# Laying the weights of a fused attention and two-MLP kernel out differently, matrix by matrix

## The reference

```python
# q, k, v: (1, 6016, 256); tau = 1
qn = q / (norm(q, axis=1) + 1e-06);  kn = k / (norm(k, axis=1) + 1e-06)
s = kn.transpose(0, 2, 1) @ qn / tau           # (1, 256, 256)
a = softmax(s, axis=-1)
x = (v @ a).reshape(6016, 256)
# first MLP, 1536 hidden units
g = x @ w_gate;  val = x @ w_val               # (256, 1536) each
x = (g * sigmoid(g) * val) @ w_out             # (1536, 256)
# second MLP, 2048 hidden units
h = x @ w_in2                                  # (256, 2048)
out = (h * clip(h + 3, 0, 6) / 6) @ w_out2     # (2048, 256)
```

## Time and profile before

| what | value |
|---|---|
| median of 2 runs | 1173.93 us (1173.82 to 1174.04) |
| the profiled execution's own time | 1172.61 us |
| its span in the profile | 1170.8 us |
| granted TensorE clock, mean | 0.996 of full speed |
| PE busy / PEld busy | 1156.0 / 972.5 us |
| VectorE / ScalarE / GpSimd busy | 718.0 / 286.7 / 80.6 us |

### The profile page before, as it was taken

How to read it: one execution, slowest core, us unless ns; L and a number is a source line. 1 busy time by engine, 2 the same in 40 slices (tenths; PEclk the granted TensorE clock), 3 DMA queues, 4 the chain that set the end, 5 groups by cost and what they waited for, 6 DMA issues and landing times.

```text
span 1170.8 us, 14739 instructions
## 1 busy us (share of the span) xinstructions
PE 1156.0 (99%) x5274; PEld 972.5 (83%) x5274; DVE 718.0 (61%) x1162; ACT 286.7 (24%) x456; POOL 80.6 (7%) x47
## 2 busy tenths in 40 slices
PE   8899999999999999999999999999999999999998
PEld 7788888888888888888888888888888888888998
DVE  5788664574575485475476466466557447548555
ACT  7551221212221222122122122122122222212121
POOL 5766000000000000000000000000000000000000
PEclk9899999999999999999999999999999999999999
DMA  9723011002002002002002001000200200100100
GB/s 342 241 91 90 1 18 18 0 0 36 0 0 36 0 0 36 0 0 36 0 0 36 0 0 23 13 0 1 35 0 0 36 0 0 32 0 0 18 2 14
DMA packets 108111, 33.76 MB, mean 29 GB/s; under 512 B 98624, under 2 KB 102464, under 8 KB 108096
## 3 DMA queue, kind: packets, MB, share of 16 engines
q1 hardware_dynamic: 107952, 33.56, 11.6%
q10 hardware_dynamic: 144, 0.00, 0.0%
HBM read 27.39 MB, written 6.16 MB: 29 GB/s over the span
## 4 chain that ended last, share of the span: by engine, by line
PE 97%; issue 1%; DVE 1%; POOL 0%; ACT 0%; POOLq 0%; DVEq 0%; ACTq 0%
PE psum L690 33%; PE psum L667 32%; PE psum L678 22%; PE psum L702 5%; PE psum L567 3%; PE psum L652 1%; PE psum L562 0%; DVE diag_q L455 0%; POOL qk_parts L298 0%; DVE norms L449 0%; PE psum L611 0%; DVE act_out L522 0%; PE psum L621 0%; DVE prod L509 0%; PE psum L615 0%
## 5 line engine op out<-in xcount | busy, mean ns | idle before, releaser
L690 PE MATMUL psum<-prod,down_w 128*128 128x512 f32 (+1 forms) x1728 | 426.8, 384 | 0.0
L690 PEld LDWEIGHTS psum<-prod,down_w 128*128 128x128 f32 x1728 | 322.5, 188 | 61.8
L678 PE MATMUL psum<-yT,up_w 128*128 128x512 f32 (+1 forms) x1152 | 281.4, 385 | 0.0
L678 PEld LDWEIGHTS psum<-yT,up_w 128*128 128x128 f32 x1152 | 215.0, 188 | 41.3
L522 DVE TENSOR_TENSOR act_out<-psum,act_out 128x512 f32<-128x512 f32 (+1 forms) x144 | 97.9, 680 | 237.4 <-PE psum L667 207.0
L667 PE MATMUL psum<-vT,gate_w 128*128 128x512 f32 (+1 forms) x864 | 215.6, 385 | 0.1
L667 PE MATMUL psum<-vT,val_w 128*128 128x512 f32 (+1 forms) x864 | 215.3, 384 | 0.0
L667 PEld LDWEIGHTS psum<-vT,gate_w 128*128 128x128 f32 x864 | 161.2, 188 | 31.7 <-DVE act_out L522 0.8
L667 PEld LDWEIGHTS psum<-vT,val_w 128*128 128x128 f32 x864 | 161.3, 188 | 30.9
L386 ACT ACTIVATE act_out<-psum 128x512 f32<-128x512 f32 (+1 forms) x144 | 85.2, 591 | 394.4 <-PE psum L667 370.8
L535 DVE SCALAR_TENSOR_TENSOR act_out<-act_out,psum 128x512 f32<-128x512 f32 (+1 forms) x192 | 129.0, 672 | 76.8 <-ACT act_out L394 76.7
(11 more groups left out here) (68 smaller groups left out, 355.0 us busy)
## 6 DMA issues: line engine op xcount, KB each, us to landing
qk<-in_q SPq DMA_DIRECT2D x11, 512.0 KB, 4.6
qk<-in_k SPq DMA_DIRECT2D x11, 512.0 KB, 5.9
v_in<-in_v SPq DMA_DIRECT2D x44, 128.0 KB, 3.4
out<-out_sb SPq DMA_DIRECT2D x44, 128.0 KB, 2.5
w_stage<-in_moe_w_out SPq DMA_DIRECT2D x7, 512.0 KB, 3.8
w_stage<-in_moe_w_in SPq DMA_DIRECT2D x4, 512.0 KB, 3.7
raw_up<-in_moe_w_gate SPq DMA_DIRECT2D x3, 512.0 KB, 6.8
raw_up<-in_moe_w_val SPq DMA_DIRECT2D x3, 512.0 KB, 7.6
```

What stands on the lines that cost most here:

```text
L678: end = mm(HID[j % 4][:, 0:n], up2_w[:, part, b, j * P:(j + 1) * P], yT[:, m, b, 0:n], start=(part, m, b) == (0, 0, 0), stop=(part, m, b) ...
L690: end = mm(banks[h][:, 0:n], w[:, part, j, h * P:(h + 1) * P], prod[:, c % 4, m, 0:n], start=j == 0 and (part, m) == PASSES[0], stop=False)
```

## The change

Where the operands of TensorE lie in memory changes, and nothing of what is computed. Tensors keep their sizes in whole multiples of 512 words, apart from the room that the offsets take.

- **Backward tokens in the first MLP.** `up` streams `vT` from the last token to the first, so the hidden units come out in reverse token order; `down` and `finish` of the first MLP stream `prod` backwards too, which puts the tokens in order again.
- **Unit blocks with a stride of 16 in `up2`.** Block j no longer is columns 128j to 128j + 127 of `up2_w` but every 16th column from j on, so each weight load reads 128 words that lie 64 bytes apart. `w_out2` is read as "(p j) c" to match. Since a block now needs columns of all four pieces, TensorE waits once for the last piece of `up2_w` before the first block, in place of a wait at every fourth block.
- **Offsets.** `val_w` begins 16 bytes later, `down_w` 64 bytes later. `down2_w` begins 16 bytes later, is laid out with one half of the channels behind the other, and the second half stands 30 words further, so it is 8 bytes off a multiple of 16.

```diff
+        def moved(name, words, by):
+            return sb(name, [P, -(-(words + by) // BANK) * BANK], fp32r)[:, by:by + words]
...
-        val_w = sb("val_w", [P, 2, KC, F1], fp32r)
+        val_w = moved("val_w", 2 * KC * F1, 4).rearrange("p (m k f) -> p m k f", m=2, k=KC)
...
-        down_w = sb("down_w", [P, 2, J1, C], fp32r)
+        down_w = moved("down_w", 2 * J1 * C, 16).rearrange("p (m j c) -> p m j c", m=2, j=J1)
         up2_w = sb("up2_w", [P, 2, KC, F2], fp32r)
-        down2_w = sb("down2_w", [P, 2, J2, C], fp32r)
+        down2_w = moved("down2_w", KC * (2 * J2 * P + 30), 4).rearrange("p (h x) -> p h x", h=KC)
...
+        def down2(part, blocks, h):
+            return down2_w[:, h, 0:2 * J2 * P].rearrange("p h (m j c) -> p h m j c", m=2, c=P)[:, :, part, blocks, :]
...
+        def down2_pieces(w):
+            view = w.rearrange("(p j) c -> p j c", j=J2)
+            return [(view[:, j:j + 4, :], [down2(part, slice(j, j + 4), slice(0, KC)) for part in range(2)], 4,
+                     lambda ap: ap.rearrange("p j (h c) -> p h j c", c=P)) for j in range(0, J2, 4)]
...
-                            end = mm(HID[(2 * j + g) % 4][:, 0:n], w[:, part, b, j * P:(j + 1) * P], vT[:, m, b, 0:n],
+                            end = mm(HID[(2 * j + g) % 4][:, 0:n], w[:, part, b, j * P:(j + 1) * P],
+                                     vT[:, m, b, 0:n][:, ::-1],
...
-                    end = mm(HID[j % 4][:, 0:n], up2_w[:, part, b, j * P:(j + 1) * P], yT[:, m, b, 0:n],
+                    end = mm(HID[j % 4][:, 0:n], up2_w[:, part, b, j::J2], yT[:, m, b, 0:n],
...
+            def down_block(w, part, j, h):
+                return w[:, part, j, h * P:(h + 1) * P] if w is down_w else down2(part, j, slice(h, h + 1))[:, 0]
+
+            def tokens(w, c, m, n):
+                return prod[:, c % 4, m, 0:n][:, ::-1] if w is down_w else prod[:, c % 4, m, 0:n]
...
-                        end = mm(banks[h][:, 0:n], w[:, part, j, h * P:(h + 1) * P], prod[:, c % 4, m, 0:n],
+                        end = mm(banks[h][:, 0:n], down_block(w, part, j, h), tokens(w, c, m, n),
...
-                pe.wait_ge(w_split, MLP2_AT + 1)
+                pe.wait_ge(w_split, MLP2_AT + 2 * (J2 // 4) - 1)
...
-                        if j % 4 == 0:
-                            pe.wait_ge(w_split, MLP2_AT + 2 * (j // 4) + 1)
```

More of the change, by code:

```diff
@@ L88, in attention_mlp_mlp_kernel @@
         gate_w = sb("gate_w", [P, 2, KC, F1], fp32r)
-        val_w = sb("val_w", [P, 2, KC, F1], fp32r)
+        val_w = moved("val_w", 2 * KC * F1, 4).rearrange("p (m k f) -> p m k f", m=2, k=KC)
         with ExitStack() as early:
             raw_up = sb("raw_up", [P, 2, KC, F1], fp32, early)
+            first_pad = sb("first_pad", [P, BANK], fp32, early)
             first_up = sb("first_up", [P, 2, 2, KC, F1], fp32r, early)
-        down_w = sb("down_w", [P, 2, J1, C], fp32r)
+        down_w = moved("down_w", 2 * J1 * C, 16).rearrange("p (m j c) -> p m j c", m=2, j=J1)
         up2_w = sb("up2_w", [P, 2, KC, F2], fp32r)
-        down2_w = sb("down2_w", [P, 2, J2, C], fp32r)
+        down2_w = moved("down2_w", KC * (2 * J2 * P + 30), 4).rearrange("p (h x) -> p h x", h=KC)
         w_stage = sb("w_stage", [P, 2, 4 * C])
@@ L194, in up_pieces @@
             step = 4 * C // KC
-            return [(view[:, :, n:n + step], dst[:, :, :, n:n + step], KC) for n in range(0, width, step)]
+            return [(view[:, :, n:n + step], [dst[:, part, :, n:n + step] for part in range(2)], KC, lambda ap: ap)
+                    for n in range(0, width, step)]
         def down_pieces(w, dst, blocks):
             view = w.rearrange("(j p) c -> p j c", p=P)
-            return [(view[:, j:j + 4, :], dst[:, :, j:j + 4, :], 4) for j in range(0, blocks, 4)]
+            return [(view[:, j:j + 4, :], [dst[:, part, j:j + 4, :] for part in range(2)], 4, lambda ap: ap)
+                    for j in range(0, blocks, 4)]
+        def down2_pieces(w):
+            view = w.rearrange("(p j) c -> p j c", j=J2)
+            return [(view[:, j:j + 4, :], [down2(part, slice(j, j + 4), slice(0, KC)) for part in range(2)], 4,
+                     lambda ap: ap.rearrange("p j (h c) -> p h j c", c=P)) for j in range(0, J2, 4)]
         PIECES = down_pieces(w_out, down_w, J1)
         MLP2_AT = len(PIECES)
-        second = zip(up_pieces(w_in2, up2_w, F2), down_pieces(w_out2, down2_w, J2))
+        second = zip(up_pieces(w_in2, up2_w, F2), down2_pieces(w_out2))
         PIECES += [piece for pair in second for piece in pair]
@@ L262, in _ @@
             load_v(v_full[0], BANK)
-            for n, (src, _, _) in enumerate(PIECES):
+            for n, (src, _, _, _) in enumerate(PIECES):
                 if n >= 2:
@@ L313, in _ @@
             pool.wait_ge(up_split, 2)
-            for n, (_, dst, _) in enumerate(PIECES):
+            for n, (_, (high, lo), _, read) in enumerate(PIECES):
                 if n == MLP2_AT:
@@ L317, in _ @@
                 pool.wait_ge(w_loaded[n % 2], 16 * (n // 2 + 1))
-                nc.gpsimd.tensor_copy(dst[:, 0], staged(n)).then_inc(w_high, 1)
+                nc.gpsimd.tensor_copy(high, read(staged(n))).then_inc(w_high, 1)
                 pool.wait_ge(w_high, n + 1)
-                nc.gpsimd.tensor_tensor(dst[:, 1], staged(n), dst[:, 0].bitcast(fp32),
-                                        ALU.subtract).then_inc(w_split, 1)
+                nc.gpsimd.tensor_tensor(lo, read(staged(n)), high.bitcast(fp32), ALU.subtract).then_inc(w_split, 1)
         @block.scalar
@@ L701, in finish @@
                         pe.wait_ge(prod_ready, t * JJ + (c + k + 3))
-                    end = mm(banks[h][:, 0:n], w[:, part, j + k, h * P:(h + 1) * P], prod[:, (c + k) % 4, m, 0:n],
+                    end = mm(banks[h][:, 0:n], down_block(w, part, j + k, h), tokens(w, c + k, m, n),
                              start=False, stop=k == 1 and (part, m) == PASSES[-1])
```

## The result

The changed kernel takes 1211.3 us (2 runs, 1211.29 to 1211.32) against 1173.93 us: 1.0318 times as long, 95% interval 1.0274 to 1.0363. That is slower by more than 2%, where a change too small to tell from none was forecast. The time lies in the stated range of 1168 to 1304 us, but by luck: that range reached so far up only to hold loads of three times the length, which did not come, and the forecast's own range ended at 1186 us.

A forecast was written before the change was run, and what follows sets the result against it. TensorE, going gaplessly from matmul to matmul at 226.7 ns, was taken as the bound; 1172.6 + 0 + 1 + 0 + 0 = 1173.6 us profiled, 1174.9 against the median, so 1175 us predicted, range 1168 to 1304 us (the forecast's own 1168 to 1186).

The forecast's parts named there:

- loads of three times the length: In `up2`, strided weight loads at 321 ns would outlast the stream: 129 us more, 1304 us in all.
- The cost of the moved wait: TensorE's wait before `up2` for the last `up2_w` piece: expected 0, the piece being ready 22.1 us ahead.
- I take zero: First MLP's 2592 backward matmuls: no cost, as 16 bytes serve four columns in either direction.
- first rival: Backward streams of the first MLP run at half pace: 542 us more, 1717 us in all; chance 0.13.
- third rival: Many small costs: 5 to 10 ns at each backward stream's start, 13 to 26 us, about 1200 us; chance 0.03.
- The strided load takes 1.69 times as long: `up2` weight loads: VectorE's measured strided-read ratio put on the contiguous 107 ns gives 181 ns; 2 us at most, 1 taken.
- the fixed 13.3 ns: Part of each 226.7 ns matmul step that does not grow with columns; 512 columns take the other 213.5 ns.
- The price given for twice: Strided loads of double length: covered by 512 columns, 96 x 53 ns = 5.1 us in the last tile.
- second rival: Strided `up2` loads outlast their cover, above twice the contiguous length: 1304 to 1426 us; a collision about 105 us; chance 0.17.
- Covered, so no cost in 11 tiles: Strided `up2` loads of 181 ns stay below the 213.5 ns stream of 512 columns: 0 in 11 tiles.
- I take 0: Shifted `val_w`, `down_w`, `down2_w`: same 16-byte groups, 33 for 32 in one half, covered; 1.7 us if uncovered.
- The mark that was set for backward streams: Sign of a wrong forecast: 12 matmuls of a first MLP taking over 2.8 us.

## Where the prediction held and where it failed, step by step

**The frame held.** TensorE bounded the kernel before and after, no engine came into its way, and the growth came from longer steps between matmuls, all but some 0.6 us of the lead-in. The cost of the moved wait stayed at nothing: GpSimd ended the last piece of `up2_w` at 103.8 us, and TensorE came to `up2` at 127.5. The timeline of GpSimd in the changed kernel:

```profile
101.34 2.43 POOL L336 TENSOR_TENSOR up_w<-w_stage,up_w 128x1024 fp32r<-128x1024 f32 x1
```

**"I take zero" for the backward tokens** is the first step that failed. The reason, four words to each 16 bytes in either direction, speaks against the half pace of the first rival, and nothing like it came. It does not exclude a small cost, and there is one: 6.7 ns (1.44 us in 216) on each of 2376 matmuls and 0.7 to 0.9 us in the last tile, 16.6 us measured alone. It is an even one: the mean over an MLP was the same in every full tile but the first of all five kernels with backward tokens, 50.39 to 50.41 us, and 6.7 ns is what 16 columns take at 0.417 ns. The third rival priced 5 to 10 ns a matmul and had 3 of 100. It was nearest in kind and size, and its 13 to 26 us hold the 16.6. Its place, the start of each stream, is not shown: with 384 columns, where as many streams start, the cost was 0.5 to 0.9 us in 216 matmuls, 2 to 4 ns each. The estimate should have asked what a stream without cover pays for any small thing, times 2592.

**"The strided load takes 1.69 times as long"** was mis-sized. The recorded load grew by 114 ns, and in the last tile, where it is bare, the step of 225 ns leaves 212 ns for it, twice the contiguous 107 (an estimate: 225 less the fixed 13.3 ns). The price given for twice, 96 x 53 = 5.1 us, is what the last tile paid (5.1 us). As to the size, VectorE's ratio was no guide to TensorE's, and with a stride of 4 the same estimate gives 220 ns, more than the 213.5 of the cover: there the second rival's condition was met, by a little.

What the Trainium skill says of 16-byte lines (Advanced Engine Details and Errata, section SBUF Cachelines) agrees with the recorded loads of this case: one hit per line made them 302 ns (stride of 16) and 311 ns (4) long, two hits with a stride of 2 kept them at 193 against 188 ns.

**"Covered, so no cost in 11 tiles"** is the step that failed most. It took the load for something that runs beside the stream and matters only once it is longer. The stride of 2 refutes that: a load recorded with 193 ns, covered with 384 columns at next to no cost, and 233 ns a step of `up2` with 512. The full tiles paid 13.9 us for the stride alone. The second rival named a collision of load and stream and was nearer in kind, but priced it at 105 us.

**"I take 0" for the offsets** counted how many 16-byte groups a block touches. By that count 16, 64 and 128 bytes are free and 8 bytes cost a little. Measured: 8 bytes, 256 bytes and, as far as it shows, 16 bytes are free, 128 bytes dear, and 64 bytes too in the one run that has them (there beside 16 on `val_w`). What counts is the place of a block of weights, by itself or against the tokens streamed beside it, and a shift by 256 bytes changed nothing. In the kernel before, all blocks of weights began at multiples of 512 bytes from where the streams begin, so no row of it could show this.

The two independent read ports that the Trainium skill gives TensorE (SBUF — State Buffer, the table under "The single rule") were used against a collision. The measurement decides otherwise as to the time: here the place and the pattern of loads that end well within the stream changed the step by 4 to 7 ns, so that stream and load are not independent in time, whatever couples them.

**The sum.** 233.3 ns in the first MLP and 234.6 in the second, against 226.7 forecast, 32.6 us in 11 tiles, and 5.8 us in the last against 1 forecast. The mark that was set for backward streams, 12 matmuls in over 2.8 us, stood where a cost of this size just reaches it: they took 2 x 1.40 = 2.80 us in the timeline above. And of the third rival's 1188 to 1201 us about seven tenths, not a third, lie within 2% of the kernel before.

**What stays open.** That load and stream meet in the memory is one explanation of the cost of place and of the stride of 2, but no run shows the meeting itself, and short loads, which should meet less, disturbed forward streams in place by 4 and 5 ns. What adds to the stride of 16 in full tiles beyond the length of its load is not known. Whether the place of the weights counts by itself or against the tokens was not told apart. The 233.3 ns of the backward stream hung neither on the place of the weights (0, 16, 64, 128 bytes) nor on the load's length, in five kernels; that it is a cost of the stream itself is the simplest reading, and why it then absorbs the cost of the offsets was not settled. That the half at 136 bytes is what makes the layout of `down2_w` dear is argued from the run with 128 bytes and was not tried by itself.

No version tried beats the kernel before, and no MLP of a full tile got under 226.7 ns a step as a mean.

## What to carry to other kernels

Where TensorE goes from matmul to matmul without a gap, a layout of its operands is a change of every step: ask for the price in nanoseconds per matmul, not whether a load is covered. Begin the blocks of weights and the tokens beside them at the same place within 256 bytes, which was free where all of them stood so (the kernel before, and all tensors 16 bytes later); weights 256 bytes later were free too. Load weights contiguously: two words of each 16 bytes kept the load short and still cost 8.7 us. Price a reversal on every matmul that streams it; whether it is cheaper where a tensor is written once was not tried. And when two parts of a change act on the same step, time them together: here they cost 37 us together and 58 apart.

## What the runs showed of the hardware that was not expected

- A 512-column fp32r stream read backwards steps by 233.3 ns on the mean where the forward one steps by 226.7, in each of five kernels, with weights at 0, 16, 64 and 128 bytes and with loads of 128 and of 40 columns beside it.
- Weights moved by 128 bytes cost 5.7 ns a step, by 256 bytes or 8 bytes nothing, and 16 bytes on all tensors nothing.
- A weight load of 128 words with a stride of 2 is recorded as hardly longer (193 against 188 ns), yet steps of `up2` beside it take 233 ns in full tiles. With a stride of 4 or 16 it is recorded with 311 or 302 ns.
- A disturbed step disturbs its neighbours: matmuls whose operands had not moved took 224 to 236 ns among moved ones, and single steps of 224 ns are shorter than any of the kernel before.
- A weight load of 40 columns in place of 128 made the forward steps longer, 232.0 and 230.6 ns.
- With 384 columns less of this shows: with weights 128 bytes off the last tile kept its 4.25 us for 24 matmuls and paid 0.5 us in 192, 2.6 ns each where full tiles paid 5.7, and a backward stream cost 2 to 4 ns a matmul where full tiles paid 6.7.
